# The last product of the second batch as seven products of quarters: a three-stage kernel on one core

## The chip, the cores and the metric

One core of a Trainium2 chip runs the whole program. The time is that of the device in microseconds, median of several runs. The engines named below are PE (TensorE, matrix products; a matmul is preceded by a load of its 128x128 weights), DVE (VectorE), ACT (ScalarE), POOL (GpSimd) and SP, which here only issues transfers.

## The reference, cut to what matters

```python
x = attention(q, k, v)                     # 2 batches x 768 tokens, 8 heads of 64: x is 1536 x 512
out = sum(p[:, e] * (relu(x @ w1[e]) @ w2[e]) for e in range(4))   # d_ff 1024
a, b = out @ moe2_w1, out @ moe2_w2        # 512 -> 1024 each
h = a * b @ moe2_w3                        # 1024 -> 1024
y = h @ moe2_w_out                         # 1024 -> 512
```

All is fp32 and the result must be near fp32. Since `(a*b) @ w3 @ w_out = (a*b) @ (w3 @ w_out)`, the kernel makes the folded weights `w3 @ w_out` (1024 x 512) once on the chip and keeps them in a tensor `folded` in device memory.

## The kernel before, in words

Every fp32 factor is split into a high part (rounded to the matmul's format) and a low part (the rest), and one product of 128 inputs takes three matmuls: high*high, high*low, low*high (`hi_lo_products`, L47 to L52). ACT makes the high parts by a copy with conversion, DVE or POOL the low parts by a subtraction.

Most large products are done with seven products of quarters in place of eight (a fast scheme with 2x2 blocks). The weights have quarters A11, A12, A22 and sums S1 to S4; the tokens have quarters B11, B21, B22 and sums T1 to T4, each with a high and a low part. The seven products are named `product1` to `product7` after their order in the scheme; PE issues them in the order 1, 4 and 3 of the group before, 6, 5, 2, 7. Results gather in three PSUM banks per group; DVE adds between them (`add_u2`, `add_u3_c22`, `add_c21`, `add_c12`), and ACT saves the first product (`snap`). A result C has four quarters: 11, 21, 12, 22. A group makes 128 output channels of both halves for 2 halves of 384 tokens each: 7 products x 2 blocks of 128 inputs x 3 matmuls = 42 matmuls over 384 columns.

The order of the program is: folding of the weights, attention of both batches, first batch (four experts, then the gated stage, then the output rows `y`), and the second batch (the same with other code).

In the second batch an expert is 4 up groups (`product1` to `product7`) and then two down groups (`down_group`), each of 7 products x 4 blocks x 3 = 84 matmuls over 384 columns. Their weights come from device memory into `raw`, POOL makes their sums (`down_sums`: `down_s1_s3`, `down_s2_s4`), ACT the high parts in `ah` (`down_high`) and POOL the low parts in `al` (`down_low`, called in sixteen parts by `parts_low`, the order of which is `DOWN_PARTS`). `ah` and `al` are a ring of three slots: up groups and down pieces take slots in turn, so the first down piece can only be split once the third last up group is done with its slot (a wait on `p3`).

The gated stage of a batch (`gated`) has 8 groups. DVE multiplies the two halves (`m_made`), ACT makes the high part in `hh` (`gated_high`) and DVE the low part in `hl` (`gated_low`). Then `y_step` multiplies by the folded weights: tokens are the stationary side (128 tokens), the weights `w2h`, `w2l` move (512 channels). Six rows of 128 tokens, 8 blocks of inputs, 3 matmuls each; in the second batch the last row is done in two halves of 256 channels (`y_last`). ACT copies a row out of PSUM and issues its transfer (`y_row`, `y_last_row`). The folded weights for it come in four pieces of 512 KB (`last`), of which ACT and POOL make both parts (`out_high`, `out_low`, 1024 wide).

At the start of the second batch's gated stage the four sums T1 to T4 of its tokens are made by DVE in two portions of 384 columns (`portion_t1` to `portion_t4`), and their low parts for the second portion by DVE too (`portion_low`), the others by POOL. The sums, and these low parts, read two operands from SBUF; the sums between products read one from PSUM.

In the first batch's first expert `expert_vector` makes the low parts of group 0's quarter 12 and group 1's quarter 11 between `group_tail` of group 0 and that of group 1. In the attention of the second batch `WindowAttention.vector` copies a finished output of four units from PSUM (`outputs`, L559) ahead of the copy of the transposed probabilities (`pt`, L610).

Of the kernel before, what the change touches and what calls it, by code (L numbers as in the profile page):

```python
# [17 lines left out]
F32 = mybir.dt.float32  # L18
# [6 lines left out]
P = 128  # L25
# [418 lines left out]
class WindowAttention:  # L444
# [151 lines left out]
    def vector(self, dve, c):  # L596
# [260 lines left out]
DRAINS = (11, 22, 21, 12)  # L857


class Dense:  # L860

# [23 lines left out]
    def __init__(self, nc, sem, lay, bank, weights, folded, gates_dram, x_dram, x_stored, out, fold, g_stored):  # L885
# [28 lines left out]
        self.rows = [sb("rows", DM, at=4 * s * DM) for s in range(2)]  # L914

# [34 lines left out]
    def pieces():  # L950
# [10 lines left out]
        order += [("down", n) for n in range(2 * DOWNS * E)]  # L961
        order += [("last", 4 + j) for j in range(4)]
# [17 lines left out]

    def wait_raw(self, eng, kind, n):
        m = self.at(kind, n)
        eng.wait_ge(self.raw_loaded[self.place(m)], 16 * len(self.uses(m)))
# [14 lines left out]
    def load_piece(self, sp, m):  # L998
# [5 lines left out]
        if kind == "last":  # L1004
# [64 lines left out]

    def load_splits(self, sp, *groups):  # L1070
        for p in range(len(LOADS)):
            for i in groups:
                self.load_split(sp, i, p)

    def sync(self, sp):
# [24 lines left out]
        i0, m = UPS + KH * E, self.at("last", 4)  # L1100
        for f in range(3, 6):
            self.load_splits(sp, i0 + f)
        self.load_piece(sp, m + 2)
        self.load_splits(sp, i0 + 6)
        self.load_piece(sp, m + 3)
        self.load_splits(sp, i0 + 7)
        for s in range(2):
            sp.wait_ge(self.y_stored[s], 16 * (B * ROWS_OUT // 2 + s))
# [15 lines left out]
    def slot_down(n):  # L1124
        e, j = divmod(n, 2 * DOWNS)
        return (UPS + PER_EXPERT * e + KH + j + 2) % 3
# [114 lines left out]
    def down_high(self, act, n, p):  # L1241
        src, to = self.down_part(n, p)
        e, j = divmod(n, 2 * DOWNS)
        if j < 2 * DOWNS - 1:
            act.wait_ge(self.p3, UPS + KH * e + j + 2)
# [177 lines left out]
    def bank_free(self, pe, i, c):  # L1423
# [8 lines left out]
        elif c == 21:  # L1432
            pe.wait_ge(self.c21_made, i + 1)
        elif c != 22:
            pe.wait_ge(self.m_low[{11: 0, 12: 1}[c]], self.m_count(i) + 1)
# [88 lines left out]

    def down_group(self, pe, j, p, ks=range(KH)):
# [4 lines left out]
        if 0 in ks:  # L1530
            if start:
                self.bank_free(pe, UPS + KH * e + 2 + d, c)
# [5 lines left out]
        for k in ks:  # L1538
            i, n = UPS + KH * e + k, 2 * j + k // 2
            s = self.slot_down(n)  # L1540
            pe.wait_ge(self.dn_low, self.part_count(n, [a in part for part in PARTS].index(True)))
            if b == T4:
                pe.wait_ge(self.t4_low, KH * e + k + 1)
            elif b >= T1:
                pe.wait_ge(self.t_low, self.low_count(i, b))
            else:
                pe.wait_ge(self.h_low[{B11: 11, B21: 21, B22: 22}[b]], self.h_count(i) + 1)
# [6 lines left out]
    def second_expert(self, pe, e):  # L1554
        i0 = UPS + KH * e
        for i in range(i0, i0 + KH):
# [9 lines left out]
            if i < i0 + KH - 1:  # L1566
                self.product1(pe, i + 1)
        j = DOWNS * e
        self.down_group(pe, j, 1, (0, 1))
        self.product4(pe, i0 + 3)  # L1570
        self.product3(pe, i0 + 3)
# [78 lines left out]
    def y_last(self, pe, t, half):  # L1650

        r, n = ROWS_OUT - 1, PIECE // 2
        for k in range(KF):
            c = slice(k * S + r * P, k * S + (r + 1) * P)
            d = slice(k * PIECE + half * n, k * PIECE + (half + 1) * n)
            last = hi_lo_products(self.nc, self.bank[4 + half][:, 0:n], (self.hh[:, c], self.hl[:, c]),
                                  (self.w2h[:, d], self.w2l[:, d]), k == 0, k == KF - 1)
        last.then_inc(self.y_done, 1)

    Y = (6, 0, 1, 2, 3, 4)  # L1660

    def gated(self, pe, t):
# [42 lines left out]
        if t == 0:  # L1705
            pe.wait_ge(self.drained, 8 * E)
        else:
            pe.wait_ge(self.x_added, 8 * E)
# [13 lines left out]
        for r in range(3, ROWS_OUT - t):  # L1722
            for k in range(KF):
                self.y_step(pe, t, r, k)
        if t == B - 1:
            self.bank_free(pe, i0 + KF - 1, 12)
            for half in range(2):
                self.y_last(pe, t, half)
# [74 lines left out]
    def down_snap(self, act, j):  # L1803
        e, d = divmod(j, DOWNS)
        act.wait_ge(self.dn_product, self.dn_count(j, 1))
        act.wait_ge(self.t_low, self.low_count(UPS + KH * e + 2 + d, T3))
# [37 lines left out]

    def second_gated_scalar(self, act):
        i0 = UPS + KH * E
# [6 lines left out]
        self.gated_high(act, 1, 0)  # L1853
        for f in range(2, KF):
            self.snap(act, i0 + f)
            self.gated_high(act, 1, f - 1)
            if f in (2, 3, 5, 6):
                self.out_high(act, "last", 2 + f - f // 4)
        self.gated_high(act, 1, KF - 1)
# [57 lines left out]
    def y_row(self, act, t, r):  # L1917
# [6 lines left out]
        act.dma_start(self.out[n * P:(n + 1) * P, :], self.rows[n % 2][:, :]).then_inc(self.y_stored[n % 2], 16)  # L1924

    def y_last_row(self, act, half):
        m, n = B * ROWS_OUT - 1, PIECE // 2
        c = slice(half * n, (half + 1) * n)
        act.wait_ge(self.y_done, m + 1 + half)
        if half == 0:  # L1930
            act.wait_ge(self.y_stored[m % 2], 16 * (m // 2))
        self.nc.scalar.activation(self.rows[m % 2][:, c], self.bank[4 + half][:, 0:n], ACT.Copy).then_inc(self.y_read, 1)
        act.wait_ge(self.y_read, m + 1 + half)
        act.dma_start(self.out[m * P:(m + 1) * P, c], self.rows[m % 2][:, c]).then_inc(self.y_stored[m % 2], 16)

    def scalar(self, act):
        for t in range(B):
# [8 lines left out]
            for r in range(ROWS_OUT):  # L1946
                if t == 0:
                    if r == 0:
# [773 lines left out]
```

## Time and profile before

| what | value |
|---|---|
| median of 3 runs | 798.39 us (797.92 to 800.03) |
| time of the profiled execution | 798.14 us |
| span of its profile | 796.6 us |
| granted TensorE clock, mean | 0.999 |
| PE busy | 788.8 us, 99% |
| DVE, ACT, POOL busy | 58%, 42%, 63% |

The span is what the trace covers; the time has 1.5 us more around it. Busy time of an engine counts each instruction from start to end, and matmuls overlap, so a busy PE need not be working at its best pace: the distance of their starts is the pace.

### The profile page before, as it was taken

To read this page: it belongs to the slowest core of one execution; us is meant where nothing else is said; L and a number is where in the kernel's file an instruction comes from. 1 tells how busy PE (TensorE), PEld (TensorE's weight loads), DVE (VectorE), ACT (ScalarE), POOL (GpSimd) and SP (SyncE) were. 2 spreads that over 40 slices of the span, in tenths; PEclk is the share of its full clock that TensorE was granted. 3 is DMA by queue.
4 is the path that set the end of the run, shared out by engine and by line. 5 is a ranking of instruction groups with operands and counts; after the bars stand their busy time and mean duration, and the time that the engine had idled before them with its cause. 6 is when DMAs were issued, how large, how long until landed. Compare 5 with 4: busy or idle time off the path is not lost.

```text
span 796.6 us, 13813 instructions
## 1 busy us (share of the span) xinstructions
PE 788.8 (99%) x4702; PEld 746.8 (94%) x4702; DVE 465.4 (58%) x1019; ACT 331.2 (42%) x706; POOL 501.8 (63%) x461
## 2 busy tenths in 40 slices
PE   9999999999999999999999999999999999999997
PEld 8777778999999999999999899999999999999986
DVE  6896687613533633624866338459568478786620
ACT  5576785422431531522434337327227137333210
POOL 3589898694683774757596528948838839922200
PEclk9999999999999999999999999999999999999999
DMA  8943565864564544645299722482582571569301
GB/s 299 371 140 117 191 229 196 359 256 173 198 237 165 201 186 178 218 153 224 96 337 382 269 68 99 150 276 76 166 280 70 168 276 54 175 215 331 127 28 56
DMA packets 49707, 155.18 MB, mean 195 GB/s; under 512 B 5968, under 2 KB 7264, under 8 KB 49632
## 3 DMA queue, kind: packets, MB, share of 16 engines
q1 hardware_dynamic: 45248, 145.67, 51.0%
q10 hardware_dynamic: 4320, 8.52, 3.0%
q8 instruction: 43, 0.70, 0.4%
q0 software_dynamic: 64, 0.03, 0.1%
q14 instruction: 32, 0.26, 0.1%
HBM read 103.31 MB, written 50.88 MB: 194 GB/s over the span
## 4 chain that ended last, share of the span: by engine, by line
PE 98%; DVE 1%; ACT 0%; issue 0%; DVEq 0%; ACTq 0%
PE bank L50 30%; PE bank L52 29%; PE bank L51 29%; PE bank L652 3%; PE bank L623 3%; PE bank L633 3%; PE bank L243 1%; PE bank L257 0%; ACT pr L520 0%; DVE hl L2123 0%; DVE pt L610 0%; DVE x_stage L559 0%; ACT pt L537 0%; DVE bank L2118 0%; ACT hh L1771 0%
## 5 line engine op out<-in xcount | busy, mean ns | idle before, releaser
L50 PE MATMUL bank<-bh,ah 128*128 128x384 f32 x672 | 225.2, 335 | 0.6 <-DVE parts L2089 0.6
L52 PE MATMUL bank<-bh,al 128*128 128x384 f32 x672 | 224.5, 334 | 0.0
L51 PE MATMUL bank<-bl,ah 128*128 128x384 f32 x672 | 224.5, 334 | 0.0
L50 PEld LDWEIGHTS bank<-bh,ah 128*128 128x128 f32 x672 | 126.2, 188 | 1.8 <-DVE parts L2089 1.2
L51 PEld LDWEIGHTS bank<-bl,ah 128*128 128x128 f32 x672 | 126.2, 188 | 0.1
L52 PEld LDWEIGHTS bank<-bh,al 128*128 128x128 f32 x672 | 126.2, 188 | 0.0
L1268 POOL TENSOR_TENSOR w2l<-raw,w2h 128x1024 fp32r<-128x1024 f32 x24 | 57.9, 2415 | 89.3 <-ACT w2h L1263 88.9
L50 PE MATMUL bank<-hh,w2h 128*128 128x384 f32 x256 | 85.5, 334 | 0.0
L51 PE MATMUL bank<-hl,w2h 128*128 128x384 f32 x256 | 85.5, 334 | 0.0
L52 PE MATMUL bank<-hh,w2l 128*128 128x384 f32 x256 | 85.5, 334 | 0.0
L1187 POOL TENSOR_TENSOR al<-raw,ah 128x512 fp32r<-128x512 f32 x48 | 62.1, 1314 | 28.6 <-ACT ah L1167 28.3
L52 PE MATMUL bank<-sh,al 128*128 128x384 f32 x224 | 74.9, 334 | 0.0
L50 PE MATMUL bank<-sh,ah 128*128 128x384 f32 x224 | 74.9, 334 | 0.0
L51 PE MATMUL bank<-sl,ah 128*128 128x384 f32 x224 | 74.8, 334 | 0.0
L1751 ACT ACTIVATE parts<-bank 128x384 f32<-128x384 f32 x48 | 23.5, 489 | 109.0 <-PE bank L52 103.5
L1257 POOL TENSOR_TENSOR al<-raw,ah 128x512 fp32r<-128x512 f32 (+1 forms) x48 | 57.6, 1219 | 17.6 <-ACT ah L1251 17.6
L1998 POOL TENSOR_TENSOR sl<-b_sum,sh 128x384 fp32r<-128x384 f32 x32 | 32.0, 1024 | 45.9 <-ACT sh L1801 45.9
L513 POOL TENSOR_TENSOR pr<-pr,rden 128x512 f32<-128x512 f32 (+1 forms) x48 | 45.8, 975 | 10.8 <-DVE rden L589 10.8
L2146 DVE TENSOR_TENSOR bank<-bank,gate 128x384 f32<-128x384 f32 x24 | 13.4, 560 | 65.9 <-PE bank L52 65.9
L2123 DVE SCALAR_TENSOR_TENSOR hl<-bank,hh 128x384 fp32r<-128x384 f32 x64 | 35.1, 550 | 24.7 <-ACT hh L1760 23.6
L51 PEld LDWEIGHTS bank<-hl,w2h 128*128 128x128 f32 x256 | 48.1, 188 | 0.0
L50 PEld LDWEIGHTS bank<-hh,w2h 128*128 128x128 f32 x256 | 48.1, 188 | 0.0
(165 smaller groups left out, 1655.2 us busy)
## 6 DMA issues: line engine op xcount, KB each, us to landing
raw<-weights SPq DMA_DIRECT2D x56, 512.0 KB, 3.6
splits<-ah SPq DMA_DIRECT2D x24, 896.0 KB, 4.2
splits<-al SPq DMA_DIRECT2D x24, 896.0 KB, 6.2
ah<-splits SPq DMA_DIRECT2D x48, 256.0 KB, 3.5
al<-splits SPq DMA_DIRECT2D x48, 256.0 KB, 4.4
ah<-splits SPq DMA_DIRECT2D x24, 384.0 KB, 4.8
al<-splits SPq DMA_DIRECT2D x24, 384.0 KB, 5.8
k<-k SPq DMA_DIRECT2D x8, 704.0 KB, 6.6
```

The lines of the kernel that those rows point to most:

```text
L50: nc.tensor.matmul(out, wh, xh, start=start, stop=False, skip_group_check=adds_on)
L51: nc.tensor.matmul(out, wh, xl, start=False, stop=False, skip_group_check=adds_on)
L52: return nc.tensor.matmul(out, wl, xh, start=False, stop=stop, skip_group_check=adds_on)
L513: self.nc.gpsimd.tensor_tensor(probs, probs, scale, ALU.mult).then_inc(self.normed, 1)
L623: last = self.nc.tensor.matmul(self.scores_of(u, h), self.q[s][head, i * P:(i + 1) * P], self.k[s][head, key0:key0 + self.width(u)], start ...
L633: last = self.nc.tensor.transpose(self.ps_t[u % 2][:, cols], self.pr[u % NS][:, cols], self.setup.ident[:, :])
L652: last = self.nc.tensor.matmul(out, self.v[s][:, t * P + D * h:t * P + D * (h + 1)], self.pt[u % 2][:, col:col + P], start=m == 0, stop=m ...
L1187: last = nc.gpsimd.tensor_tensor(self.al[s][:, c], self.raw_of("up", g)[:, c], self.ah[s][:, c].bitcast(F32), ALU.subtract)
L1257: self.nc.gpsimd.tensor_tensor(self.al[s][:, to], src, self.ah[s][:, to].bitcast(F32), ALU.subtract).then_inc(self.dn_low, 1)
L1268: self.nc.gpsimd.tensor_tensor(self.w2l[:, c], self.raw_of(kind, n)[:, :], self.w2h[:, c].bitcast(F32), ALU.subtract).then_inc(self.w2_low, 1)
L1998: self.nc.gpsimd.tensor_tensor(self.sl[b][k][:, :], self.t_raw(i, b), self.sh[b][k][:, :].bitcast(F32), ALU.subtract).then_inc(self.t_low, 1)
L2123: self.nc.vector.scalar_tensor_tensor(self.hidden(self.hl, i, c), self.c_of(i, c), 0.0, self.hidden(self.hh, i, c).bitcast(F32), ALU.max, ...
```

## The change

- **The last product of the second batch.** In place of the six rows of `y` (120 matmuls of 512 columns and 48 of 256) there are two more down groups (E = 4 as "fifth expert"): `down_groups(pe, E, ...)`, with the channels of the output as rows. The stationary side is now the folded weights, the moving side the gated tokens in 384 columns. The four quarters are written to `out` by channels, and the host turns that half.
- **The weights.** The four pieces of 512 KB of folded weights are now read as four quarters each (blocks of 128 columns, so runs of 512 bytes), summed by POOL (`down_sums`), split by ACT (`down_high`) and POOL (`parts_low`, sixteen parts) as in an expert.
- **The tokens.** Groups are taken in pairs: the even group gives quarters 11 and 12, the odd one 21 and 22. ACT keeps 11, DVE makes T1 to T4 (`pair_sum`), ACT the high parts (`pair_high`), POOL the low parts (`gated_h11_low`, `pair_lows`), DVE those of 21 and 22.
- **The end.** `copy_end` and `down_sum` write the quarters to SBUF, SP stores eight of them (`store_end`).
- **Two moves.** In the first expert two low parts are now made after group 1's `add_u3_c22`. In the second batch's attention the output's copy comes behind that of `pt`.

```diff
@@ WindowAttention.vector
-        if 0 <= u < UNITS and (u + 2) % PER_OUT == 0:
-            self.outputs(dve, u // PER_OUT)
+        g = u // PER_OUT
+        put_out = 0 <= u < UNITS and (u + 2) % PER_OUT == 0
+        if put_out and g < OUTS0:
+            self.outputs(dve, g)
...
             nc.vector.tensor_copy(self.pt[1][:, :], self.ps_t[1][:, :]).then_inc(self.odd_copied, 1)
+        if put_out and g >= OUTS0:
+            self.outputs(dve, g)
@@ load_piece
+        if self.transfers(m) > 1:
+            d, a = divmod(n % (2 * DOWNS), 2)
+            blocks = self.folded.rearrange("r (p k m d c) -> r p k m d c", p=KH, k=2, m=2, d=DOWNS)
+            for q, (half, k) in enumerate(((0, 0), (0, 1), (1, 1), (1, 0))):
+                to = dst[:, q * QUART:(q + 1) * QUART].rearrange("r (p c) -> r p c", p=2)
+                sp.dma_start(to, blocks[:, 2 * a:2 * a + 2, k, half, d, :]).then_inc(done, 16)
@@ sync
-        for f in range(3, 6):
+        for f in range(3, KF):
             self.load_splits(sp, i0 + f)
         self.load_piece(sp, m + 2)
-        self.load_splits(sp, i0 + 6)
         self.load_piece(sp, m + 3)
-        self.load_splits(sp, i0 + 7)
+        for d in range(DOWNS):
+            for c in ENDS:
+                self.store_end(sp, d, c)
@@ bank_free, second batch
+            p, second = divmod(self.m_count(i) - KF, 2)
+            if not second:
+                pe.wait_ge(*((self.h_high[11], self.pair_h(p)) if c == 11 else (self.t_made, self.pair_count(p, T1))))
+            else:
+                pe.wait_ge(self.h_low[21 if c == 11 else 22], self.pair_h(p))
+                pe.wait_ge(self.t_made, self.pair_count(p, T4 if c == 11 else T2))
@@ gated
+        if t:
+            self.down_groups(pe, E, i0 + KF - 1)
+            return
@@ second_gated_scalar
+        for q in range(KF):
+            p = q // 2
+            if 1 <= q < KF - 1:
+                self.snap(act, i0 + q + 1)
+            if q == KF - 1:
+                for m, k in DOWN_PARTS[4:8]:
+                    self.down_high(act, n0 + m, k)
+            self.gated_kept(act, q)
+            if q == KF - 1:
+                self.down_snap(act, DOWNS * E)
+            if q % 2 == 0:
+                if p:
+                    self.pair_high(act, p - 1, T3)
+                self.pair_high(act, p, T1)
+            else:
+                self.gated_h22(act, p)
+                for b in self.pair_sums(p)[1:3 if q < KF - 1 else 4]:
+                    self.pair_high(act, p, b)
+            for m, k in {KF - 2: DOWN_PARTS[0:4], KF - 1: DOWN_PARTS[8:]}.get(q, ()):
+                self.down_high(act, n0 + m, k)
+                if (m, k) == (2, 2):
+                    self.down_snap(act, DOWNS * E + 1)
+        for d in range(DOWNS):
+            self.copy_end(act, d)
@@ second_gated_gpsimd
+        for b, k in ((B11, 0), (B21, 0), (T1, 0), (T2, 0), (B22, 0), (T3, 0), (B11, 1), (B22, 1), (T4, 0), (B21, 1)):
+            self.portion_low(pool, self.nc.gpsimd, b, k)
+        for n in range(2):
+            self.down_sums(pool, n0 + n)
+        for p in range(KH - 1):
+            self.gated_h11_low(pool, p)
+            self.pair_lows(pool, p, self.pair_sums(p))
+        p = KH - 1
+        self.parts_low(pool, E, 0, 2)
+        self.gated_h11_low(pool, p)
+        self.pair_lows(pool, p, (T1,))
+        self.parts_low(pool, E, 2, 8)
+        self.down_s1_s3(pool, n0 + 2)
+        self.pair_lows(pool, p, (T2, T3, T4))
+        self.down_s2_s4(pool, n0 + 2)
+        self.parts_low(pool, E, 8, 11)
+        self.down_sums(pool, n0 + 3)
+        self.parts_low(pool, E, 11, 16)
@@ group_tail
         self.add_u3_c22(dve, i)
+        if i == 1:
+            self.h_split_low(dve, 0, 12)
+            self.h_split_low(dve, 1, 11)
         self.add_c21(dve, i)
@@ second_gated_group (new)
+        def rest():
+            if q and q % 2 == 0:
+                self.pair_h_low(dve, p - 1, 22)
+                self.pair_sum(dve, p - 1, T3)
+        self.gated_sums(dve, 1, q, rest)
+        self.gated_product(dve, 1, q)
+        if q % 2 == 0:
+            self.pair_sum(dve, p, T1)
+            return
+        self.pair_h_low(dve, p, 21)
+        self.pair_sum(dve, p, T2)
+        if q == KF - 1:
+            self.pair_sum(dve, p, T3)
+            self.pair_sum(dve, p, T4)
+            self.pair_h_low(dve, p, 22)
+        else:
+            self.pair_sum(dve, p, T4)
```

## Rows read from the trace of the kernel before

**Rows 1.** The page: busy us, share of the span, instructions of the engines

```profile
PE 788.8 (99%) x4702; PEld 746.8 (94%) x4702; DVE 465.4 (58%) x1019; ACT 331.2 (42%) x706; POOL 501.8 (63%) x461
```

**Rows 2.** Waits of PE: for whom, us in total, times, longest

```profile
PE bank L50 <- DVE parts L2089: 0.6, 1, 0.6
PE bank L652 <- DVE pt L610: 0.5, 1, 0.5
```

**Rows 3.** Timeline of PE, first and last matmul of `y`: start us, us

```profile
755.80 0.39 PE L50 MATMUL bank<-w2h,hh 128*128 128x512 f32 x1
...
790.78 0.28 PE L52 MATMUL bank<-w2h,hl 128*128 128x256 f32 x1
```

**Rows 4.** Timeline of ACT and its queue at the end

```profile
791.10 0.38 ACT L1932 ACTIVATE rows<-bank 128x256 f32<-128x256 f32 x1 [2.49 <-PE bank L52]
791.51 0.34 ACTq L1934 DMA_DIRECT2D out<-rows  x1
```

**Rows 5.** Timeline of DVE, gated groups 6 and 7 (starts)

```profile
748.71 0.56 DVE L2089 TENSOR_TENSOR parts<-bank,parts 128x384 f32<-128x384 f32 x1 [1.62 <-PE bank L52]
...
751.46 0.57 DVE L2348 TENSOR_TENSOR bank<-bank,parts 128x384 f32<-128x384 f32 x1
...
752.88 0.56 DVE L2073 TENSOR_TENSOR parts<-bank,parts 128x384 f32<-128x384 f32 x1 [0.39 <-PE bank L52]
...
753.81 0.56 DVE L2356 TENSOR_TENSOR bank<-bank,parts 128x384 f32<-128x384 f32 x1
756.00 0.56 DVE L2089 TENSOR_TENSOR parts<-bank,parts 128x384 f32<-128x384 f32 x1 [1.63 <-PE bank L52]
```

**Rows 6.** Timeline of ACT: an expert's high parts, and a gated one

```profile
657.05 1.15 ACT L1251 ACTIVATE ah<-raw 128x512 fp32r<-128x512 f32 x2
...
665.95 0.53 ACT L1801 ACTIVATE sh<-b_sum 128x384 fp32r<-128x384 f32 x1 [0.47 <-DVE b_sum L2175]
...
752.06 0.49 ACT L1783 ACTIVATE hh<-bank 128x384 fp32r<-128x384 f32 x1 [1.81 <-DVE bank L2348]
```

**Rows 7.** Timeline of POOL in the last expert

```profile
657.76 2.55 POOL L1257 TENSOR_TENSOR al<-raw,ah 128x512 fp32r<-128x512 f32 x2 [3.18 <-ACT ah L1251]
660.26 2.00 POOL L1998 TENSOR_TENSOR sl<-b_sum,sh 128x384 fp32r<-128x384 f32 x2
...
672.96 0.75 POOL L1221 TENSOR_TENSOR a_sum<-raw 128x256 f32<-128x256 f32 x1
673.79 0.74 POOL L1223 TENSOR_TENSOR raw<-raw 128x256 f32<-128x256 f32 x1
```

**Rows 8.** Timeline of DVE, start of the gated stage: T2's second portion, `u2`

```profile
703.22 0.56 DVE L1356 TENSOR_TENSOR b_sum<-x 128x384 f32<-128x384 f32 x1
...
706.47 0.55 DVE L2073 TENSOR_TENSOR parts<-bank,parts 128x384 f32<-128x384 f32 x1
```

**Rows 9.** Timeline of POOL, its last low parts before the gated stage

```profile
696.57 6.20 POOL L1343 TENSOR_TENSOR bl<-x,bh 128x384 fp32r<-128x384 f32 x6
```

**Rows 10.** Timelines of POOL and DVE where both read SBUF

```profile
438.31 2.68 POOL L1268 TENSOR_TENSOR w2l<-raw,w2h 128x1024 fp32r<-128x1024 f32 x1 [4.46 <-ACT w2h L1263]
438.77 3.04 DVE L1295 TENSOR_TENSOR b_sum<-x 128x768 f32<-128x768 f32 x1
...
694.15 0.62 DVE L1362 TENSOR_TENSOR x<-b_sum,x 128x384 f32<-128x384 f32 x1
```

**Rows 11.** Timeline of DVE ahead of PE's two waits

```profile
110.62 0.69 DVE L559 COPY x_stage<-bank 128x512 f32<-128x512 f32 x1
...
138.33 0.55 DVE L2089 TENSOR_TENSOR parts<-bank,parts 128x384 f32<-128x384 f32 x1
```

**Rows 12.** The page, transfers by issue: count, KB each, median us to landing

```profile
raw<-folded SPq DMA_DIRECT2D x8, 512.0 KB, 6.3
```

**Rows 13.** Timeline of SP's queue before the gated stage

```profile
689.47 1.89 SPq L1005 DMA_DIRECT2D raw<-folded  x2
691.41 0.43 SPq L1067 DMA_DIRECT2D ah<-splits  x1
```

More of the change, by code:

```diff
@@ L914, in __init__ @@
         self.rows = [sb("rows", DM, at=4 * s * DM) for s in range(2)]
+        self.ends = {c: [nc.alloc_sbuf_tensor_at(f"end{c}_{d}", [P, TT], F32, offset=lay["bh"] + 4 * TT * (DOWNS * m + d))
+                         for d in range(DOWNS)] for m, c in enumerate(ENDS)}
+        self.out_rows = out[0:S * DM].rearrange("(n c) -> n c", c=DM)
+        self.out_channels = out[S * DM:].rearrange("(c n) -> c n", n=S)
         self.raw_loaded = [sem(f"raw_loaded{s}") for s in range(3)]
@@ L960, in pieces @@
         order += [("last", j) for j in range(4)]
-        order += [("down", n) for n in range(2 * DOWNS * E)]
-        order += [("last", 4 + j) for j in range(4)]
+        order += [("down", n) for n in range(2 * DOWNS * (E + 1))]
         return order
@@ L979, in raw_of, with transfers @@
         return self.raw[self.place(self.at(kind, n))]
+    def transfers(self, m):
+        kind, n = self.pieces()[m]
+        return 4 if kind == "down" and n >= 2 * DOWNS * E else 1
     def wait_raw(self, eng, kind, n):
         m = self.at(kind, n)
-        eng.wait_ge(self.raw_loaded[self.place(m)], 16 * len(self.uses(m)))
+        eng.wait_ge(self.raw_loaded[self.place(m)], 16 * sum(self.transfers(j) for j in self.uses(m)))
     @staticmethod
@@ L1068, in load_split, with store_end @@
                          self.splits[g * P:(g + 1) * P, src]).then_inc(self.split_loaded[s][p], 16)
+    def store_end(self, sp, d, c):
+        m = len(ENDS) * d + ENDS.index(c)
+        if c == 11:
+            sp.wait_ge(self.y_read, ROWS_OUT + d + 1)
+        else:
+            sp.wait_ge(self.dn_sum, self.sum_count(DOWNS * E + d, f"c{c}"))
+        row, half = d + (DOWNS if c > 20 else 0), 0 if c % 10 == 1 else 1
+        if m < 2:
+            sp.wait_ge(self.y_stored[m], 16 * (ROWS_OUT // 2))
+        sp.dma_start(self.out_channels[row * P:(row + 1) * P, half * TT:(half + 1) * TT],
+                     self.ends[c][d][:, :]).then_inc(self.y_stored[m % 2], 16)
     def load_splits(self, sp, *groups):
@@ L1648, in y_step @@
             last.then_inc(self.y_done, 1)
[L1650 to L1658, printed above, removed]
     Y = (6, 0, 1, 2, 3, 4)
@@ L1721, in gated @@
         self.bank_free(pe, i0 + KF - 1, 21)
-        for r in range(3, ROWS_OUT - t):
+        for r in range(3, ROWS_OUT):
             for k in range(KF):
                 self.y_step(pe, t, r, k)
[L1725 to L1728, printed above, removed]
     def tensor(self, pe):
@@ L1852, in second_gated_scalar @@
             self.portion_high(act, b, 1)
[L1853 to L1859, printed above, removed]
+        for q in range(KF):
[12 more added lines that the diff above has]
+                self.pair_high(act, p, T1)
+            else:
+                self.gated_h22(act, p)
[7 more added lines that the diff above has]
+            self.copy_end(act, d)
     def expert_scalar(self, act, n):
@@ L1923, in y_row @@
         act.wait_ge(self.y_read, n + 1)
[L1924 to L1934, printed above, removed]
+        act.dma_start(self.out_rows[n * P:(n + 1) * P, :], self.rows[n % 2][:, :]).then_inc(self.y_stored[n % 2], 16)
     def scalar(self, act):
@@ L2043, in gpsimd @@
             self.second_expert_gpsimd(pool, e)
-        for b, k in ((B11, 0), (B21, 0), (T1, 0), (T2, 0), (B22, 0), (T3, 0), (B11, 1), (B22, 1), (T4, 0), (B21, 1)):
-            self.portion_low(pool, on, b, k)
-        for j in range(4, 8):
-            self.out_low(pool, "last", j)
+        self.second_gated_gpsimd(pool)
     def after_down(self, dve, i, what):
@@ L2291, in second_gated_vector @@
         self.portion_low(dve, on, T4, 1)
-        for f in range(KF):
-            self.gated_group(dve, 1, f)
+        for q in range(KF):
+            self.second_gated_group(dve, q)
+        for j in (DOWNS * E, DOWNS * E + 1):
+            for what in DOWN_SUMS:
+                self.down_sum(dve, j, what)
     def expert_vector(self, dve, n):
@@ L2340, in gated_group @@
             self.add_u2(dve, i + 1)
[L2341 to L2344 removed]
+        between()
         self.add_c21(dve, i)
```

202 lines of the change are left out of this document (150 added, 52 removed).

## The prediction, made before the changed kernel was run

> **What bounds the kernel now.** I read the page's busy times first: PE is busy for 788.8 of 796.6 us [rows 1]. Then PE's waits: beside the first one after the launch there are two, of 0.6 and 0.5 us [rows 2]. So PE is the bound nearly everywhere, and it is fed by three engines that finish just in time. Two things can then change the time: how many columns PE streams, and whether some engine comes too late. For the pace I take the distance between two `u3` sums of neighbouring gated groups, 748.71 and 756.00 [rows 5]: 7.28 us for 42 matmuls, 0.1733 us for each with 384 columns (its busy 0.33 us overlaps the next). One product of 6 matmuls takes 1.04 us, a down group 84 x 0.1733 = 14.56 us. The timelines of the three other engines give the rest.
>
> **The matmuls.** `y` runs from 755.80 to the last start at 790.78 [rows 3], that is 35.1 us with that matmul's own slot of about 0.12. In it lie the last `product4` and `product3` (12 x 0.1733 = 2.1 us), which stay. So 33.0 us go and 2 x 14.56 = 29.1 us come: **-3.9 us**. The saving is one eighth of the products, and a little less as a matmul of 384 columns pays more per column.
>
> **The two moves.** At 138.93 PE waits for a `u3` that started at 138.33, behind two low parts that go behind it now [rows 2, 11]: 0.6 us. At 111.96 it waits for a copy of `pt` that stood behind an output's copy of 0.69 us, started at 110.62 [rows 2, 11]: 0.5 us. The other moved copies hide now and after, as PE waits for none of them. Together **-1.1 us**; bounds 0 (another engine is late next) and -1.3.
>
> **The tokens' parts.** A pair gives DVE four sums and two low parts in place of four low parts, at about 0.5 us distance: 0.5 us more a group, and DVE sits idle for 1.62 us before each `u3` [rows 5]. `product1` of the group after next now waits for T4 of an odd group. From the middle row of a group: `m` of half 12 starts 5.10 us after its `u3` [rows 5], one place earlier without the low part before it, 4.6; ACT's high part of 22 follows 0.6 us behind (751.46 to 752.06 [rows 5, 6]) and takes 0.49; then T2 and T4, each 0.6: T4 is done near 6.9 us after `u3`, `product1` is due near 7.1. Zero, with little reserve; at most 0.2 us in three places.
>
> **The start of the gated stage.** POOL's low parts end at 696.57 + 6.20 = 702.8 [rows 9], and POOL rests afterwards. Now `down_sums` of two pieces comes here at once: eight sums of 0.75 us at 0.8 us distance [rows 7], until 709 or later. In the same time DVE makes T2, the low parts of T1 and T2, T3, T4 and the low part of T3, from 703.22 on, and then `u2` at 706.47 [rows 8]: six instructions with two operands in SBUF. The trace shows what such an instruction does beside POOL: one of 768 columns took 3.04 us from 438.77, until POOL's own instruction had ended (438.31 + 2.68 = 440.99) and 0.85 us more [rows 10]. It waits for the instruction that POOL is in. Another, at 694.15, took 0.62 us beside a busy POOL [rows 10], so the wait can be near nothing if it falls between two. If each of the six waits for one sum, less what overlaps, that is 0.65 us each, 3.9 us: `u2` ends at 706.47 + 0.55 + 3.9 = 710.9. PE's need: the gated stage starts 54 products (324 matmuls, 56.2 us) before 755.80, at 699.6, and `product7` of group 0 is its ninth product, due at 707.96. PE waits **+3.0 us**, part of it earlier, at the second halves of products 5 and 6, for the low parts of T1 and T2. Bounds: 0 (0.1 us each, the margin is 0.9) and 6 x 0.75 - 0.9 = +3.6. I take the value near the upper end, as the long wait is the one with POOL surely inside an instruction.
>
> The Trainium skill says the same of the cause (GPSIMD Engine Reference, Specifications): POOL shares its SBUF interfaces with VectorE, and instructions of VectorE with two SBUF inputs contend. By that rule the sum includes this term; without it, it would be 3.0 us less. The wait of 2.2 us in the row agrees.
>
> **The last pair and the weights.** This is the dear part. I count from PE's start of group 7, 755.80 - 7.28 = 748.52, which is zero here.
> - DVE: `u2` of group 7 starts at 4.36 [rows 5], the product `m` 12 of group 6 one place earlier than before, 4.83 instead of 5.29 [rows 5], T1 of the last pair at 5.49, done at 6.05.
> - ACT: the high part of T1 from 6.09, and only behind it the first part of the folded weights, from 6.5 (0.43 us distance). In an expert this part was made before the sums of a group two groups earlier, and hid.
> - POOL starts 0.7 us after the high part's start (657.05 to 657.76 [rows 6, 7]), at 7.3, and needs 1.3 us. The first down product, due at 7.28, starts at 8.6: PE waits **1.35 us**.
> - POOL's list then: second part 1.25, low part of 11 and T1 0.98 each, parts three and four 1.25 + 0.7, and the first part of the second piece, done at 15.0 ([rows 7] for 512, 384 and 256 columns: 2.55 for two, 2.00 for two, 0.75 each). PE needs it for blocks 2 and 3 of `down_group` 1, which follow the first two blocks, `product4` and `product3`, at 8.6 + 3.1 = 11.75: PE waits **3.3 us**.
> - Then 1.25 + 1.25 + 0.7 for three parts, 1.5 for S1 and S3 of the third piece, 1.0 for T2: T2 of the last pair is low at 20.65. PE needs it for the last block of product 6, at 16.05 + 3.65 = 19.7: **1.0 us**.
> Behind that POOL keeps ahead: the third piece's first part is ready at 25.3 and due at 29.5; the fourth's S parts at 33 and due at 34.2, the tightest. T2's own sum isn't late: ACT's `down_snap` waits for product 1 until 16.4, the high part of 22 stands behind it, T2 comes at 17.3 and its high part at 18.4, before POOL takes it at 19.6. Together **+5.6 us**. Bounds: 5 (DVE's chain earlier) and 7.5, if T3's sum of the pair before, with two SBUF operands, or POOL's instructions contend.
>
> **The transfers.** A folded piece is now four transfers of runs of 512 bytes. Third piece: issued when the second part is low (9.8), needed at 18.1; with 6.3 us to landing [rows 12] and three more issues of 0.43 [rows 13] it lands at 17.4: 0. Before the gated stage the two pieces at 689.47 are followed by the split weights of group 1 from 691.41 [rows 13], due at 700.2; 1.4 us later they still land if landing stays near 6 us. Cover 2.5 us; if it is gone PE waits up to 4. I take 0. By the Trainium skill (DMA: Bandwidth & Descriptors, Specifications) 512 bytes still reach line rate, which leaves the sum as it is; nothing in this trace shows such runs alone.
>
> **The end.** Before: last matmul's start, ACT's copy 0.32 us later, issue at 791.51, end at 796.6, so 5.8 us [rows 3, 4]. After: DVE's sum of 384 columns (0.56 for 0.38), SP's issue: **+0.3 us**; from 0 to 1. The earlier seven stores lie beside the products.
>
> **Sum.** 796.6 - 3.9 - 1.1 + 3.0 + 5.6 + 0.3 = 800.5 us of span. The profiled execution has 1.5 us around it: **802.0 us**. It was 0.25 us under the median, which I let lie. A measurement tells about 0.3%, 2.4 us, from no change: 796.0 to 800.8.
>
> **Rivals.**
> - *Only the last pair is late.* The sums of POOL fall between DVE's instructions, as at 694.15, or come later than I think. 802.0 - 3.0 = 799.0, no change. For it: the one short case. Chance 0.25.
> - *The scheme pays as it counts.* The weights' parts for the first two pieces come before PE needs them, as in the four experts, in which PE never waits with the same POOL work and the same order of products. Then the last pair costs at most 1 us and POOL's start at most 1: 796.6 - 3.9 - 1.1 + 0.3 + 1.5 + 1.5 = 794.9. Against it: ACT's list puts these parts behind T1 of the last pair. It decides the sign if the first part is low before 7.3 and the fifth before 10.4. Chance 0.12.
> - *Runs of 512 bytes are slow.* If a piece takes twice its time to land, the third is 5 us late at POOL, and group 1's weights too: 802 + 3 = 805, up to 808. Chance 0.08.
> - *The two moves bring nothing*: 803.1; inside the likeliest one's range.
>
> **How the numbers follow.** My forecast has chance 0.55, and of its range 800 to 804 about one sixth lies under 800.8. Slower: 0.46 + 0.08 = 0.54. Same: 0.09 + 0.25 = 0.34. Faster 0.12. For 8 in 10 the range is 797.0 to 804.8.
>
> **What would show it.** PE's waits in the last 45 us: one for the first part of the weights (`al`, POOL), one of about 3 us for the fifth, one of 1 us for T2's low part. In the start: DVE's sums at 703 to 710 with 1.0 to 1.3 us in place of 0.56, and `product7` of group 0 late. Two waits of the first 140 us gone. It is wrong if POOL has the first part low before `product7` of the last group ends, if DVE's sums keep 0.56 us beside `down_sums`, or if a folded piece lands more than 8 us after its issue.

## The result, and the profile after

The changed kernel takes 802.6 us, median of 6 runs (800.54 to 803.83), against 798.74 us of the kernel before (6 runs, 797.92 to 800.03): ratio 1.0045, 95% interval 1.0028 to 1.0061. It is slower by 3.9 us by the medians, 3.6 by the ratio. The profiled execution was its fastest, 800.54 us with a span of 798.7; the other five have spans of 799.9 to 802.0. So the trace explains 2.1 us of the difference (798.7 against 796.6 us of span); what single executions add is told below.

The page of the changed kernel, busy times:

```profile
PE 786.9 (99%) x4702; PEld 747.7 (94%) x4702; DVE 479.0 (60%) x1037; ACT 341.2 (43%) x731; POOL 543.9 (68%) x509
```

PE has 1.9 us less to do, POOL 42 us more [rows 1]. Its waits, each with the releaser, the sum in us, the number and the longest; of the two of [rows 2] neither is left:

```profile
PE bank L50 <- POOL al L1297: 2.9, 1, 2.9
PE bank L50 <- issue: 2.0, 2, 1.1
PE bank L243 <- DVE blank L2780: 1.1, 1, 1.1
PE bank L50 <- DVE bl L1383: 0.9, 2, 0.6
PE bank L50 <- DVE parts L2203: 0.6, 1, 0.6
PE bank L50 <- DVE parts L2219: 0.4, 1, 0.4
PE bank L637 <- POOL pr L513: 0.2, 1, 0.2
```

The same waits in the timeline of PE, the first matmul after each. The wait in brackets is counted from the end of the matmul before, whose end overlaps the next start by 0.16; against the pace of 0.173 us from start to start the seven cost 0.8, 0.4, 0.7, 0.5, 1.0, 1.3 and 3.1 us.

```profile
703.30 0.41 PE L50 MATMUL bank<-bh,ah 128*128 128x384 f32 x1 [0.64 <-DVE bl L1383]
...
704.30 0.41 PE L50 MATMUL bank<-bh,ah 128*128 128x384 f32 x1 [0.24 <-DVE bl L1383]
...
707.72 0.45 PE L50 MATMUL bank<-bh,ah 128*128 128x384 f32 x1 [0.57 <-DVE parts L2203]
```

```profile
714.61 0.44 PE L50 MATMUL bank<-bh,ah 128*128 128x384 f32 x1 [0.37 <-DVE parts L2219]
...
720.93 0.41 PE L50 MATMUL bank<-bh,ah 128*128 128x384 f32 x1 [0.85 <-issue]
```

```profile
758.82 0.41 PE L50 MATMUL bank<-sh,ah 128*128 128x384 f32 x1 [1.12 <-issue]
...
765.10 0.45 PE L50 MATMUL bank<-sh,ah 128*128 128x384 f32 x1 [2.91 <-POOL al L1297]
...
766.06 0.52 PE L51 MATMUL bank<-sl,ah 128*128 128x384 f32 x1
766.38 0.52 PE L52 MATMUL bank<-sh,al 128*128 128x384 f32 x1
```

The last two lines show something else: behind the long wait, from 765.74 on, ten matmuls start 0.32 us from each other in place of 0.173. From 765.8 to 768.9 us the granted clock is 0.50, the lower of its two levels (1.2 GHz in place of 2.4). That costs 1.5 us.

**The start of the gated stage.** The timelines of DVE and of POOL, whose names are as in [rows 8, 9] (L1396 is T2's second portion, L1383 low parts, L2203 `u2`):

```profile
701.16 0.98 DVE L1396 TENSOR_TENSOR b_sum<-x 128x384 f32<-128x384 f32 x1
702.07 1.09 DVE L1383 TENSOR_TENSOR bl<-x,bh 128x384 fp32r<-128x384 f32 x1
703.08 1.08 DVE L1383 TENSOR_TENSOR bl<-b_sum,bh 128x384 fp32r<-128x384 f32 x1
704.08 1.08 DVE L1402 TENSOR_TENSOR x<-b_sum,x 128x384 f32<-128x384 f32 x1
705.08 1.09 DVE L1407 TENSOR_TENSOR x<-x,b_sum 128x384 f32<-128x384 f32 x1
706.10 1.09 DVE L1383 TENSOR_TENSOR bl<-x,bh 128x384 fp32r<-128x384 f32 x1
707.12 0.55 DVE L2203 TENSOR_TENSOR parts<-bank,parts 128x384 f32<-128x384 f32 x1
```

```profile
700.67 1.05 POOL L1261 TENSOR_TENSOR a_sum<-raw 128x256 f32<-128x256 f32 x1
701.80 0.94 POOL L1263 TENSOR_TENSOR raw<-raw 128x256 f32<-128x256 f32 x1
702.70 1.04 POOL L1269 TENSOR_TENSOR a_sum<-a_sum,raw 128x256 f32<-128x256 f32 x1
```

Six instructions of DVE take 0.98 to 1.09 us in place of 0.56. POOL's sums are stretched as well, to 0.93 to 1.05 us from 0.75 [rows 7], and one instruction of each starts about every 1.0 us: the two engines take turns.

**The last pair.** The timelines of ACT and POOL (L1938 on ACT is T1's high part and L2136 on POOL a low part of the sums, L1291 and L1297 the high and low parts of the folded weights, L2130 the low part of 11):

```profile
756.33 0.53 ACT L1938 ACTIVATE sh<-x 128x384 fp32r<-128x384 f32 x1 [1.25 <-DVE x L2537]
756.76 1.14 ACT L1291 ACTIVATE ah<-raw 128x512 fp32r<-128x512 f32 x2
757.80 0.92 ACT L1291 ACTIVATE ah<-a_sum 128x512 fp32r<-128x512 f32 x2
```

```profile
757.45 2.52 POOL L1297 TENSOR_TENSOR al<-raw,ah 128x512 fp32r<-128x512 f32 x2 [1.27 <-ACT ah L1291]
759.94 1.01 POOL L2130 TENSOR_TENSOR sl<-x,sh 128x384 fp32r<-128x384 f32 x1
760.91 1.00 POOL L2136 TENSOR_TENSOR sl<-x,sh 128x384 fp32r<-128x384 f32 x1
761.88 1.95 POOL L1297 TENSOR_TENSOR al<-a_sum,ah 128x512 fp32r<-128x512 f32 x2
763.79 4.42 POOL L1297 TENSOR_TENSOR al<-raw,ah 128x512 fp32r<-128x512 f32 x4
```

The first high part stands right behind that of T1. PE starts at 758.82 when POOL's first low part is done, and at 765.10 when the first of the four from 763.79 on is.

**The end.** The last matmul starts at 794.70, and DVE's last sum 0.38 us later:

```profile
795.08 0.56 DVE L2369 TENSOR_TENSOR end<-bank,parts 128x384 f32<-128x384 f32 x1 [1.53 <-PE bank L52]
```

From the last matmul's start to the end of the span it is 4.0 us, before 5.8 [rows 3, 4]. The last transfer of the kernel before, and then that of the changed one, with KB and the time from issue to landing:

```profile
out<-rows ACTq DMA_DIRECT2D x1, 128.0 KB, 1.7
```

```profile
out<-end SPq DMA_DIRECT2D x1, 192.0 KB, 2.6
```

Before, the last store lands at about 793.2 and the span ends 3.4 us later; after, it lands at about 798.3, 0.5 us before the end. So the store itself takes longer now, and what is shorter is the time behind its landing.

### The profile page after: what moved, and what is told of

It reads as the page before. It is cut to its first block and busy times, and to the rows that moved or that the text cites. A ratio compares the mean times of both kernels' runs of the same rounds, so it can differ in the third digit from the quotient of the medians.

```text
span 798.7 us, 14038 instructions
## 1 busy us (share of the span) xinstructions
PE 786.9 (99%) x4702; PEld 747.7 (94%) x4702; DVE 479.0 (60%) x1037; ACT 341.2 (43%) x731; POOL 543.9 (68%) x509
## 5 line engine op out<-in xcount | busy, mean ns | idle before, releaser
L50 PE MATMUL bank<-sh,ah 128*128 128x384 f32 x280 | 94.5, 338 | 4.0 <-POOL al L1297 2.9
L51 PE MATMUL bank<-sl,ah 128*128 128x384 f32 x280 | 94.2, 337 | 0.0
L52 PE MATMUL bank<-sh,al 128*128 128x384 f32 x280 | 94.2, 336 | 0.0
L1297 POOL TENSOR_TENSOR al<-raw,ah 128x512 fp32r<-128x512 f32 (+1 forms) x60 | 71.6, 1214 | 19.6 <-ACT ah L1291 19.6
L1308 POOL TENSOR_TENSOR w2l<-raw,w2h 128x1024 fp32r<-128x1024 f32 x20 | 48.3, 2418 | 49.9 <-ACT w2h L1303 49.5
L50 PEld LDWEIGHTS bank<-sh,ah 128*128 128x128 f32 x280 | 53.0, 189 | 4.7 <-POOL al L1297 3.2
L51 PEld LDWEIGHTS bank<-sl,ah 128*128 128x128 f32 x280 | 53.1, 190 | 0.0
L52 PEld LDWEIGHTS bank<-sh,al 128*128 128x128 f32 x280 | 53.1, 190 | 0.0
```

Source lines behind the costliest of these rows:

```text
L50: nc.tensor.matmul(out, wh, xh, start=start, stop=False, skip_group_check=adds_on)
L51: nc.tensor.matmul(out, wh, xl, start=False, stop=False, skip_group_check=adds_on)
L52: return nc.tensor.matmul(out, wl, xh, start=False, stop=stop, skip_group_check=adds_on)
L1297: self.nc.gpsimd.tensor_tensor(self.al[s][:, to], src, self.ah[s][:, to].bitcast(F32), ALU.subtract).then_inc(self.dn_low, 1)
L1308: self.nc.gpsimd.tensor_tensor(self.w2l[:, c], self.raw_of(kind, n)[:, :], self.w2h[:, c].bitcast(F32), ALU.subtract).then_inc(self.w2_low, 1)
```

## The experiments

Each kernel is timed in turn with the kernel before. To set them beside the changed kernel I use the ratios to the kernel before (802.6 is 1.0045). By their intervals the difference of two such ratios is good to some 1.5 us either way, so sizes under 2 us rest on the waits in the traces more than on the times.

**Eight idle sums in the kernel before.** This puts the suspected cause where nothing else of the change is.

```diff
             self.portion_low(pool, on, b, k)
+        self.wait_raw(pool, "last", 4)
+        for j in range(8):
+            if j:
+                pool.wait_ge(self.dn_step, 16 * E + j)
+            raw, to = self.raw_of("last", 4), slice(j % 3 * QUART, (j % 3 + 1) * QUART)
+            self.nc.gpsimd.tensor_tensor(self.a_sum[:, to], raw[:, 0:QUART], raw[:, QUART:2 * QUART],
+                                         ALU.add).then_inc(self.dn_step, 1)
```

> The kernel before with eight more sums of 256 columns on POOL right behind its low parts at the start of the gated stage; their results are not used. Nothing of the last product is changed. Theory (VectorE's instructions with two operands in SBUF wait for POOL's): VectorE's portions take 1.0 to 1.1 us in place of 0.56, PE waits 2.5 to 3 us there, the kernel is 2.5 to 3 us slower. Rival (the waits of the changed kernel at this place come from its smaller transfers or later split weights): VectorE keeps 0.56 us and the time doesn't change.

Measured: 800.42 us against 798.49, ratio 1.0021 (1.0012 to 1.0030), +1.7 us. DVE and POOL in its timelines, at the same place:

```profile
704.31 0.98 DVE L1356 TENSOR_TENSOR b_sum<-x 128x384 f32<-128x384 f32 x1
705.21 1.09 DVE L1343 TENSOR_TENSOR bl<-x,bh 128x384 fp32r<-128x384 f32 x1
```

```profile
703.81 7.10 POOL L2051 TENSOR_TENSOR a_sum<-raw 128x256 f32<-128x256 f32 x7
```

The instructions take the same 0.98 and 1.09 us, and PE waits before 706.45, 707.45 and 710.85 as in the changed kernel, 1.9 us against the pace. The rival falls: this happens without its transfers and its products. The size is under the 2.5 us that I had expected: the fourth wait (u3 of group 1, 0.5 us) isn't there; it belongs to something else.

**POOL's first sums later.** The converse, in the changed kernel:

```diff
+        pool.wait_ge(self.u2_made, UPS + KH * E + 1)
         for n in range(2):
             self.down_sums(pool, n0 + n)
```

> The changed kernel, but POOL begins the sums of the first two folded pieces only when u2 of gated group 0 is made. Theory: the waits for VectorE's low parts and u2 at the start of the gated stage (from start to start 0.8, 0.4, 0.7 us above the pace) and that for u3 behind it (0.5) are gone: 2.4 to 2.7 us faster than the changed kernel, some 800.1 us; the waits at the last pair stay. Rival (transfers): the waits stay where they are, 802.6 us.

Measured: 800.45 us against 798.49, ratio 1.0022 (1.0013 to 1.0031); that is 0.0023 or 1.8 us under the changed kernel. DVE's instructions are back at their length:

```profile
701.30 0.56 DVE L1396 TENSOR_TENSOR b_sum<-x 128x384 f32<-128x384 f32 x1
701.86 0.56 DVE L1383 TENSOR_TENSOR bl<-x,bh 128x384 fp32r<-128x384 f32 x1
```

The first three waits are gone, the other four are all there, the one for u3 of group 1 too, which I had forecast to go; so the gain is under the 2.4 us expected. POOL's sums cost 1.9 us at this place, by the waits, and 1.7 and 1.8 us by the times: shown from both sides.

**The weights' parts earlier.** ACT's first four high parts go to the head of its list for group 6, POOL's low parts of them ahead of T3 of the third pair, the fifth ahead of the last pair's.

```diff
+            if q == KF - 2:
+                for m, k in DOWN_PARTS[0:4]:
+                    self.down_high(act, n0 + m, k)
             if 1 <= q < KF - 1:
                 self.snap(act, i0 + q + 1)
...
         for p in range(KH - 1):
             self.gated_h11_low(pool, p)
-            self.pair_lows(pool, p, self.pair_sums(p))
+            self.pair_lows(pool, p, self.pair_sums(p)[:3])
+            if p < KH - 2:
+                self.pair_lows(pool, p, (T3,))
+        self.parts_low(pool, E, 0, 4)
+        self.pair_lows(pool, p, (T3,))
         p = KH - 1
-        self.parts_low(pool, E, 0, 2)
+        self.parts_low(pool, E, 4, 5)
         self.gated_h11_low(pool, p)
+        self.parts_low(pool, E, 5, 6)
         self.pair_lows(pool, p, (T1,))
-        self.parts_low(pool, E, 2, 8)
+        self.parts_low(pool, E, 6, 8)
```

> The changed kernel with the first four high parts of the folded weights at the head of ACT's list for group 6 in place of its end, and POOL's low parts of them ahead of T3 of the third pair, the fifth ahead of the last pair's. Theory (the parts' place in two lists makes PE wait 1.3 and 3.1 us): both waits fall under 0.5 us each, and PE's clock, which the trace shows at half speed for 3 us behind the long wait, doesn't fall: 4.5 to 6 us faster than the changed kernel, some 797.5 us. Rival (POOL has too much to do in the last 45 us, so that the wait only moves on to T2's low part and to the third and fourth piece): PE waits about as long in sum, under 2 us faster.

Measured: 797.65 us against 798.49, ratio 0.9988 (0.9979 to 0.9997), 0.0057 or 4.6 us under the changed kernel. Both waits are gone, the slow matmuls too. The one wait of PE in the last 45 us is for T2's low part, 1.9 us against the pace:

```profile
767.50 0.41 PE L50 MATMUL bank<-sh,ah 128*128 128x384 f32 x1 [1.72 <-POOL sl L2139]
```

So the waits were a matter of place in two lists. Part of their cost comes back: the third wait that I had forecast is 1.9 us here, 0.6 us more than in the next run, which has the changed kernel's lists and a full clock.

**The folded pieces in runs of 4 KB.**

```diff
-        return 4 if kind == "down" and n >= 2 * DOWNS * E else 1
+        return 1
...
+            if kind == "down" and n >= 2 * DOWNS * E:
+                a = n % (2 * DOWNS) * 2 * PIECE
+                sp.dma_start(dst[:, :], self.folded[:, a:a + 2 * PIECE]).then_inc(done, 16)
+                return
```

> The changed kernel, but a folded piece is read in one transfer with runs of 4 KB in place of four with runs of 512 bytes; the blocks then stand in other places, so the second batch's output is another one. Theory (the transfers are hidden): same waits of PE as in the changed kernel, 802 to 803 us. Rival (the small runs delay POOL or the split weights): one or more of the waits is gone or shorter, over 1 us faster.

Measured: 801.6 us against 797.94, ratio 1.0049 (1.0035 to 1.0062). Every wait of the changed kernel is there with its length, though the transfers themselves land otherwise (median 5.8 us for those of 512 KB in this run, 2.5 us for those of 128 KB in the changed kernel); the transfers are hidden. It shows one thing more. In this execution the clock stayed full, and PE met a third wait at the last pair:

```profile
759.81 0.41 PE L50 MATMUL bank<-sh,ah 128*128 128x384 f32 x1 [1.12 <-issue]
...
766.08 0.44 PE L50 MATMUL bank<-sh,ah 128*128 128x384 f32 x1 [2.91 <-POOL al L1301]
...
772.15 0.41 PE L50 MATMUL bank<-sh,ah 128*128 128x384 f32 x1 [1.12 <-POOL sl L2140]
```

The third is the one for T2's low part, 1.3 us against the pace; the trace of the next run has it too. In the changed kernel's trace the ten slow matmuls took its place: PE came later, and POOL was done. So the last pair costs 1.3 + 3.1 + 1.3 = 5.7 us with a full clock and 1.3 + 3.1 + 1.5 = 5.9 us with the slow stretch.

**The moves undone.** In the changed kernel `outputs` goes ahead of `pt`'s copy again and the two low parts ahead of `add_u3_c22`, as in the kernel before.

> The changed kernel with both moves undone. Theory (what the two moves bring, 1.6 us in the kernel before with them alone, doesn't hang on the rest): 1.6 us slower than the changed kernel, some 804.2 us. Rival (it is lost in the later waits): 802.6 us.

Measured: 803.45 us against 797.94, ratio 1.0064 (1.0050 to 1.0078): 0.0019 or 1.5 us above the changed kernel. The intervals of the two ratios overlap, so this run alone shows no difference; it agrees with the next one.

**The moves alone**, in the kernel before:

> The kernel before with the two moves alone. Theory (each move takes away the one wait that its rows show, 0.9 us from start to start of two pieces of PE's work at 111.04, of which 0.3 is work, and 0.95 for 0.17 at 137.98): 1.1 to 1.4 us faster than before. Rival (what the changed kernel's trace shows, 2.1 us gained until the gated stage, is all from the moves): 2.1 us faster. Second rival (the next engine is late in their place): no change.

Measured: 796.91 us against 798.49, ratio 0.9981 (0.9972 to 0.9990), -1.5 us. Its waits of PE are only these, so both of [rows 2] are gone and little came in their place:

```profile
PE bank L243 <- DVE blank L2581: 1.1, 1, 1.1
PE bank L637 <- POOL pr L513: 0.2, 1, 0.2
PE bank L50 <- POOL fold_mt_l L225: 0.2, 1, 0.2
PE bank L50 <- DVE fold_wo_l L220: 0.2, 1, 0.2
```

**Two waits in groups 1 to 3.** In group 3 `product6` and `product1` change places, and T1 of the first pair is made behind u3 of group 1.

```diff
-            self.product1(pe, i)
+            late = t and i == i0 + 3
+            (self.product6 if late else self.product1)(pe, i)
             self.product4(pe, i - 1)
             self.product3(pe, i - 1)
-            self.product6(pe, i)
+            (self.product1 if late else self.product6)(pe, i)
...
         def rest():
+            if q == 1:
+                self.pair_sum(dve, 0, T1)
...
         if q % 2 == 0:
-            self.pair_sum(dve, p, T1)
+            if q:
+                self.pair_sum(dve, p, T1)
```

> The changed kernel with product1 of gated group 3 behind product3 of group 2 (product6 in its place), and T1 of the first pair made behind u3 of group 1. Theory (product1 of group 3 waits 1.0 us for T4 of the first pair, as group 1's sums have one product less ahead of it than in later groups, and u3 of group 1 waits 0.5 us behind T1): both waits gone, the rest as in the changed kernel, 1.5 us faster, some 801.1 us. Rival (the 1.0 us, which the profile gives no releaser, is a load of split weights): that wait stays, 0.5 us faster.

Measured: 801.55 us against 797.94, ratio 1.0035 (1.0021 to 1.0048), 0.8 us under the changed kernel by the ratios, within their intervals, where 1.5 us was expected. The wait for u3 is gone from its trace (0.1 us is left), that ahead of group 3 is not: 1.2 us, now before `product6`. As `product6` doesn't wait for T4, this run tells nothing of T4; the S parts of group 3's weights are asked for last and were issued at 715.02 and 715.49, so `product6` in the first place probably waited for them: the median landing of the two such transfers here is 6.1 us, which gives 721.6 as an estimate, and PE starts at 721.69. That wasn't tried. A second kernel does it on DVE, with the order of the products left as it was:

```diff
-        if 0 < f < KF - 1:
+        if 0 < f < KF - 1 and not (t and f == 1):
             self.add_u2(dve, i + 1)
...
         self.gated_product(dve, 1, q)
+        if q == 1:
+            self.add_u2(dve, UPS + KH * E + 2)
```

> The changed kernel with one thing in another order: VectorE makes the second product m of gated group 1 ahead of u2 of group 2, not behind it. Theory (product1 of group 3 waits for T4 of the first pair): T4 ends some 0.5 us earlier and so does PE's wait there, 1.0 to 0.5 us. Rival (it waits for its split weights): the wait stays at 1.0 us.

Measured in one execution: 801.77 us, from which no difference of time can be read. The wait fell from 1.0 to 0.4 us against the pace. T2 and T4 end at 719.60 + 1.14 = 720.74, PE starts at 720.84; in the changed kernel it was 719.68 + 1.15 = 720.83, and 720.93. PE starts 0.10 us behind T4's end in both, and the wait shrinks as T4 comes earlier: it is T4.

**All mends together.** POOL's sums later, the parts earlier, group 3's order and T1 of the first pair as above, and for the last pair T2's low part ahead of the sums of the next weights:

```diff
-        self.down_s1_s3(pool, n0 + 2)
-        self.pair_lows(pool, p, (T2, T3, T4))
+        self.pair_lows(pool, p, (T2,))
+        self.down_s1_s3(pool, n0 + 2)
+        self.pair_lows(pool, p, (T3, T4))
```

> The changed kernel with all mends: POOL's first sums behind u2 of group 0 (2.0 us by its own run), the weights' parts earlier (4.9 us by its own run), group 3's order and T1 of the first pair (1.5 us), and T2's low part of the last pair ahead of the third piece's S1 and S3 (of 1.9 us left there, 1.5). Theory (the waits are apart from each other and add): 802.6 - 2.0 - 4.9 - 1.5 - 1.5 = 792.7 us, 0.7% faster than the kernel before and 4 us faster than that with the two moves alone. Rival (POOL becomes the bound of the last 45 us, and what is taken from one wait comes back in another): 795 us or more.

Measured: 794.82 us against 797.94, ratio 0.9960 (0.9947 to 0.9974), 3.2 us under the kernel before by the ratio. It misses the 792.7 us of the sum by 2.1 us and comes out beside the rival's 795: what was taken from one wait came back in part in another. Three waits of 0.4 to 0.6 us are left or new in its gated and last stage, 0.75, 0.6 and 0.6 us against the pace, 2.0 in all:

```profile
PE bank L50 <- DVE parts L2380: 0.6, 1, 0.6
PE bank L50 <- ACT parts L1874: 0.4, 1, 0.4
PE bank L50 <- issue: 0.4, 1, 0.4
```

The first is told under what I had not expected, the second is for ACT's `down_snap`, the third stands ahead of group 3. The last version has group 3's own order back and DVE's order of the run before:

> As the kernel with all mends, but group 3 keeps its own order of products (which put product6 where its weights or sums weren't ready) and the second product m of group 1 goes ahead of u2 of group 2. Theory: the 0.6 us that the other one waits in group 3 falls to 0.5 or less, the rest as there: 794.2 to 794.8 us. Rival (that wait is the weights' transfer): no better than 794.8 us.

Measured: 794.86 us against 798.58, ratio 0.9952 (0.9938 to 0.9966), 3.8 us under the kernel before by the ratio. The wait in group 3 fell to 0.4 us as in that run, so it wasn't the rival's transfer; but the time is no better than the rival's 794.8. By time the two versions can't be told apart, since the wait for ACT's `down_snap` of the second down group grew to 1.3 us, before 777.21: it stands behind a high part that waits for POOL's sums of the fourth piece. A version without that one wasn't tried.

## Why the prediction was right, and where it was not

802.0 us was forecast and 802.6 measured, slower as forecast. The mechanism was right in its dearest term, the last pair, and in the cause at the start of the stage; that the sum came so close is in part luck, as shown below. The terms:

| term | forecast | shown |
|---|---|---|
| matmuls | -3.9 | -3.9: a down group takes 795.08 - 780.51 = 14.57 us between its last sums |
| two moves | -1.1 | -1.5, by two pairs of runs |
| POOL's sums at the start | +3.0 | +1.9 by the waits, +1.7 and +1.8 by two runs |
| T4 of an odd group | 0, at most 0.2 | +1.0 in group 1, 0 in the others |
| u3 of group 1 | not named | +0.5 |
| last pair | +5.6 | +5.7 with a full clock (two other executions), +5.9 with the slow stretch (this one) |
| transfers | 0 | 0 |
| end | +0.3 | -1.8 in this trace |

The last pair came as it was counted from the rows, wait by wait: 1.35, 3.3 and 1.0 us forecast, 1.3, 3.1 and 1.3 measured, the third only where the clock stayed full. That the time of the first two comes back when ACT's and POOL's lists are changed, and nothing else, shows the cause.

Four terms were off in size. At the start each of six instructions of DVE was given nearly a whole sum of POOL, 0.65 us; they lost 0.42 to 0.53 us each, 3.1 us in all, and the margin of 0.9 us was free. The step "it waits for the instruction that POOL is in" was too simple: every instruction lost about the same, POOL's sums were longer too, and one of each takes 1.0 us together, where one whole instruction after the other would take 0.56 + 0.75 = 1.31 us. The step "zero, with little reserve" for T4 took its count from group 6. In group 1 only `product2` and `product7` of group 2 lie between `product6`, which DVE's `u2` waits for, and the next `product1`, and in later groups `product5` too: 1.04 us less, and that is the wait. The wait for u3 of group 1 is T1 of the first pair ahead of it on DVE. The moves brought more since I took the waits of [rows 2] and not the distance of starts, which is some 0.15 us more for each and gives 1.4 us.

The end was wrong in sign. The sum put a longer copy and SP's issue into it and took all that follows as fixed. By the profiles the last store lands 1.7 us after its issue in the three executions with the old last product, and 3.4 to 3.6 us more pass until the span ends; in the nine with the new one it lands after 2.6 to 3.8 us, and 0.4 to 0.5 us more pass. So from the last matmul's start to the end it is 5.8 to 6.1 us in the three and 4.0 to 5.2 in the nine: shorter in all of them, by less than 1.8 us in most. The engine, the queue, the size and the number of the stores changed together; which of them matters wasn't tried.

By the table alone the trace would be -3.9 - 1.5 + 1.9 + 1.5 + 5.9 - 1.8 = +2.1 us, which is the difference of the spans. That closes only by luck, as two things are left out. One is the program's first matmuls: the same matmul of the first attention (`bank<-k,q`, 64x256) starts at 41.94 us in the changed kernel's trace and at 42.72 in that of the kernel before, ahead of everything that was changed; over the twelve traces here it starts between 41.94 and 43.95. The other is that the matmul behind a wait takes some 0.1 us more than the pace, seven times. By stages: PE reaches the gated stage 2.1 us earlier (697.14 against 699.20), the stage with the first wait of the last pair is 5.1 us longer, the rest up to the last matmul 0.9 longer, the end 1.8 shorter.

So this trace is one with an early start and a short end, and the median is 2.1 us above it, where in the kernel before it is 0.6 us above the profiled execution. The five other executions have spans 1.2 to 3.3 us longer, and the two longest a mean clock of 0.994, where this one has 0.998. Over 800 us that is at most 3.2 us, less what of it lay in waits or took the place of one. Where it lay is open, as there is no trace of them. So the forecast's closeness to 0.6 us is partly terms that cancel: +1.1 too much for POOL's sums and 2.1 for the end, against 1.5 us of waits in group 1 and before group 3 that it had at nothing, and what this one trace is below the median.

## What to carry to other kernels

A stage that ran without a wait in one place needs its lists counted anew in another: the same down group, with the same work on POOL and the same order on PE, had its weights' parts earlier there than here, and waits of 1.3 and 3.1 us hung on where they stood in ACT's and POOL's lists. Fewer products pay only what is left when the last operands' parts come in time: of 3.9 us in matmuls the changed kernel kept nothing, and with the lists put in order it kept 3.2 to 3.8 us with the moves, of which the moves are 1.5. Where VectorE has instructions with two operands in SBUF that PE waits for, give POOL its work before or after, and look at the trace again: together the mends brought 2.1 us less than their sum.

## What the runs showed of the hardware that I had not expected

**The clock falls behind one wait, and not always.** After a gap of 3.25 us from start to start PE ran ten matmuls at the lower clock (granted 0.50, 0.32 us for 0.173) in the traces of the changed kernel, of the kernel with later sums, of that with T4 earlier, and nine in that of the group order. In those with runs of 4 KB and with the moves undone the gap was the same 3.25 us, and none was slow. Gaps of 0.6 to 2.05 us in the gated stage and behind it were never followed by such a stretch. What decides it at 3.25 us is open.

**What follows the last store's landing isn't fixed.** It was 3.4 to 3.6 us in three executions with the old last product and 0.4 to 0.5 us in nine with the new one, where the last store comes from another queue and is of another size. Which of these matters wasn't tried.

**POOL's instructions in a row can keep DVE out for more than one of them.** This was seen once. In the version with all mends T3 of the last pair, both operands in SBUF, took 2.90 us, while POOL ran low parts one behind the other. DVE's and POOL's timelines:

```profile
760.71 2.90 DVE L2548 TENSOR_TENSOR x<-x 128x384 f32<-128x384 f32 x1
```

```profile
759.52 2.02 POOL L1297 TENSOR_TENSOR al<-raw,ah 128x512 fp32r<-128x512 f32 x2
761.46 1.04 POOL L2140 TENSOR_TENSOR sl<-x,sh 128x384 fp32r<-128x384 f32 x1
762.43 0.76 POOL L1261 TENSOR_TENSOR a_sum<-raw 128x256 f32<-128x256 f32 x1
763.28 0.94 POOL L1263 TENSOR_TENSOR raw<-raw 128x256 f32<-128x256 f32 x1
```

It ended at 763.61, so by its usual 0.56 us it ran from about 763.05 (an estimate), inside or after the sum of 0.76 us, and had let two low parts end before. The `u2` behind it made PE wait 0.6 us. In the next version the same instruction took 0.56 us at 761.62, beside low parts of POOL as well, so it isn't so each time. Where POOL's sums depend on each other, as at the start of the gated stage, the wait was never over 0.53 us; whether that is the reason wasn't tried.
